# GpSimd makes the low parts of a weight strip, and of half of the second matrix, in one operation each

## The chip, the cores and the metric
The kernel runs on one core of one Trainium2 chip. The metric is the device time of one execution in microseconds (us), the lower the better. The core has five engines that this case speaks of: TensorE (PE) multiplies matrices, with its weight loads shown apart (PEld); VectorE (DVE), ScalarE (ACT) and GpSimd (POOL) work elementwise; SyncE (SP) here only issues DMAs. Each engine takes its own instructions in their order, and the kernel's author has set every wait between them by hand, with semaphores.

## The reference
Attention with a sliding window and four sink positions gives x (1536 tokens of 512). A first mixture of experts sends each token to one of eight experts. A second one, where this change lies, sends every token through all eight and adds them up with weights:

```python
for e in range(E):                     # E = 8, x: 1536x512, w1: 512x1024, w2: 1024x512
    h = np.maximum(x @ w1[e], 0.0)
    ye = h @ w2[e]
    out += P[:, e:e + 1] * ye
```

P are the gate's probabilities, balanced in eight rounds by rows and by columns (Sinkhorn).

## The kernel before, in words
Everything is computed in float32 to nearly full precision, though TensorE multiplies rounded numbers (fp32r). So every operand is split into a high part (rounded) and a low part (what the rounding left), and each product becomes three matmuls: high by high, high by low, low by high.

The first product of the second layer is made by Winograd's form of Strassen's scheme: the tokens' two halves and w1's rows and columns make 2x2 blocks, and seven products (P1, P6, P7, P2, P5, P4, P3, in that order) take the place of eight. For w1 this needs seven operand blocks of 256 numbers per partition: four that come from memory and sums of them. One such set of seven, 128x1792 numbers, is a *strip*. An expert has four strips (p = 0..3), kept in two buffers.

An expert's work is four *units* (u = 0..3). In a unit TensorE makes `up(e,u,0)` and `up(e,u,1)`, the first products for the two strips of the pair on one quarter of the tokens' columns (line 1995, 7 products of 6 matmuls of 384 columns each), and then `down(e,u)`, the second product (line 2020, 72 matmuls of 512 columns). Two units use the same pair of strips and the same half of w2 (`hu` = 0 or 1); here such two units are called a *half*. A half is then 2 x (up, up, down).

What the other engines do for it:

- GpSimd, for each half, in this order (`split_half`): for each of two strips four sums (lines 726 to 734), then, when ScalarE has rounded them, the low parts of the strip (line 739); then the low parts of half of w2, 128x2048 numbers in four chunks of 512 (line 746). The next strip's four sums stand behind these in its queue, and so do the next half's.
- ScalarE rounds a strip in two pieces (line 935) and w2 in four chunks (line 944). The four chunks are set between the steps of `up_evacuate` for the first up of the half: after the copy of P1's result, after the high part of block c11 (line 964), after c22's (line 970), and after c21's (line 974). Then come c12's high part (line 978) and the next up.
- VectorE (`up_finish`), for each up: u2 (line 1490), u3 (line 1497), the low part of c11, then c22 (line 1503), c21 (line 1509), the low part of c22, c12 (line 1514), and the low parts of c21 and c12. All low parts of the hidden values are line 1485; c11's reads the result bank `ps`, the other three read t_u3, t_c21 and t_u2 in SBUF. After a down it adds six output tiles to the accumulator (line 1525, reads `ps` and `acc`).

TensorE's waits inside an up: P6 of an up waits for the u2 of the up before, P4 (the sixth product) for this up's u3, P3 for its c22. A down waits for the low parts of w2 and for those of the hidden values. `up(e,u,j)` with even u waits for its strip.

At the start of the second layer the tokens' rows are read back, VectorE makes sums of them (`x2_combine`, lines 1435 to 1438, four operations a tile, all operands in SBUF), TensorE transposes, ScalarE rounds and VectorE makes the low part (line 1443, reads `ps`). During units 1 and 2 of the first expert VectorE also carries Sinkhorn's rounds (lines 1449 to 1460); lines 1451 and 1460 scale the table `mix` in SBUF, and TensorE adds up its columns (line 1958).

The loop over experts 1 to 7 is one code for all; expert 0 is written out ahead of it.

Of the kernel before, what the change touches and what calls it, by code (L numbers as in the profile page):

```python
# [8 lines left out]
ALU = mybir.AluOpType  # L9
# [9 lines left out]
def attention_moe_moe(nc, q, k, v, n_sink, window, modality_id, w_gate1, modality_bias, w1a, w2a,  # L19
# [37 lines left out]
    with ctx:  # L57
        def sem(name):
            return ctx.enter_context(nc.semaphore(name))
# [4 lines left out]
        def at(name, shape, dt, offset):  # L64
            return nc.alloc_sbuf_tensor_at(name, shape, dt, offset=BASE + offset)
# [174 lines left out]
        OPS = 7  # L240
# [10 lines left out]
        w1_raw = at("w1_raw", [PART, 2, OPS, 256], f32, R0 + 136 * KB)  # L251
        w1_lo = at("w1_lo", [PART, 2, OPS, 256], f32r, R0 + 136 * KB)
        w1_hi = at("w1_hi", [PART, 2, OPS, 256], f32r, R0 + 150 * KB)
        w2_raw = at("w2_raw", [PART, 4, DM], f32, R0 + 164 * KB)
        w2_hi = at("w2_hi", [PART, 4, DM], f32r, R0 + 172 * KB)
        w2_lo = at("w2_lo", [PART, 4, DM], f32r, R0 + 180 * KB)
# [116 lines left out]
        w1_split = sem("w1_split")  # L373
        w2_loaded = sem("w2_loaded")
        w2_rounded = sem("w2_rounded")
        w2_split = sem("w2_split")
# [202 lines left out]
        def _(pool):  # L579
# [142 lines left out]
            def split_w1(e, p):  # L722

                j, k = p % 2, e * 4 + p
                pool.wait_ge(w1_loaded[j], e * 64 + 32 * (p // 2 + 1))
                pool.tensor_tensor(w1_raw[:, j, OP_S1, :], w1_raw[:, j, OP_S3, :], w1_raw[:, j, OP_A22, :], ALU.add) \  # L726
                    .then_inc(w1_summed, 1)
                pool.tensor_tensor(w1_raw[:, j, OP_S3, :], w1_raw[:, j, OP_A11, :], w1_raw[:, j, OP_S3, :], ALU.subtract) \
                    .then_inc(w1_summed, 1)
                pool.wait_ge(w1_summed, e * 16 + (4 * p + 1))  # L730
                pool.tensor_tensor(w1_raw[:, j, OP_S2, :], w1_raw[:, j, OP_S1, :], w1_raw[:, j, OP_A11, :], ALU.subtract) \
                    .then_inc(w1_summed, 1)
                pool.wait_ge(w1_summed, e * 16 + (4 * p + 3))
                pool.tensor_tensor(w1_raw[:, j, OP_S4, :], w1_raw[:, j, OP_A12, :], w1_raw[:, j, OP_S2, :], ALU.subtract) \  # L734
                    .then_inc(w1_summed, 1)

                pool.wait_ge(w1_rounded, e * 8 + (2 * p + 2))
                for o in range(OPS):
                    last = pool.tensor_tensor(w1_lo[:, j, o, :], w1_raw[:, j, o, :], w1_hi[:, j, o, :], ALU.subtract)  # L739
                last.then_inc(w1_split, 1)  # L740

            def split_w2(e, hu):

                for c in range(4):
                    pool.wait_ge(w2_rounded, e * 8 + (4 * hu + c + 1))
                    last = pool.tensor_tensor(w2_lo[:, c, :], w2_raw[:, c, :], w2_hi[:, c, :], ALU.subtract)  # L746
                last.then_inc(w2_split, 1)

            def split_half(e, hu):
                split_w1(e, 2 * hu)  # L750
                split_w1(e, 2 * hu + 1)
                split_w2(e, hu)
# [1325 lines left out]
```

## Time and profile before
| | |
|---|---|
| median of 3 runs | 1405.94 us (1405.76 to 1407.05) |
| the profiled execution, its own time | 1408.68 us |
| its span, first to last instruction | 1406.9 us |
| PE busy | 1377.3 us, 98% |
| DVE busy | 705.2 us, 50% |
| ACT busy | 450.7 us, 32% |
| POOL busy | 411.4 us, 29% |
| mean granted TensorE clock | 0.990 of full speed |

The span is 1.8 us shorter than the time of its own execution, which holds what lies before the first and behind the last instruction. Busy times are sums over the whole program; which engine sets the end in a stage is read from what waits for what there. In the rows, a name without its number stands for all parts of a tensor: `h_lo<-t_u,h_hi` writes h2_lo from t_u2 or t_u3 and h2_hi, `w_lo` is w1_lo (128x256) or w2_lo (128x512).

### The profile page before, as it was taken

To read this page: it belongs to the slowest core of one execution; us is meant where nothing else is said; L and a number is where in the kernel's file an instruction comes from. 1 tells how busy PE (TensorE), PEld (TensorE's weight loads), DVE (VectorE), ACT (ScalarE), POOL (GpSimd) and SP (SyncE) were. 2 spreads that over 40 slices of the span, in tenths; PEclk is the share of its full clock that TensorE was granted. 3 is DMA by queue.
4 is the path that set the end of the run, shared out by engine and by line. 5 is a ranking of instruction groups with operands and counts; after the bars stand their busy time and mean duration, and the time that the engine had idled before them with its cause. 6 is when DMAs were issued, how large, how long until landed. Compare 5 with 4: busy or idle time off the path is not lost.

```text
span 1406.9 us, 21704 instructions
## 1 busy us (share of the span) xinstructions
PE 1377.3 (98%) x7527; PEld 1227.1 (87%) x7528; DVE 705.2 (50%) x1289; ACT 450.7 (32%) x867; POOL 411.4 (29%) x607
## 2 busy tenths in 40 slices
PE   8999989999799999999999999999999999999999
PEld 7999678888788888899998889999888899988888
DVE  7887572142464644444554444455444445544444
ACT  5887431242143432223131222323222222322221
POOL 2111022222430523325051432506143241605330
PEclk9999999999989999999999999999999999999999
DMA  6441352121301010101110101011101010110101
GB/s 131 90 101 44 137 212 102 45 75 38 135 31 31 30 31 31 31 31 30 45 45 30 30 30 30 30 45 45 30 30 30 30 30 32 36 48 33 30 31 59
DMA packets 95519, 73.85 MB, mean 52 GB/s; under 512 B 43248, under 2 KB 76016, under 8 KB 95472
## 3 DMA queue, kind: packets, MB, share of 16 engines
q1 hardware_dynamic: 90016, 65.32, 15.1%
q0 software_dynamic: 2416, 7.87, 1.7%
q8 instruction: 28, 0.46, 0.1%
q10 hardware_dynamic: 3040, 0.06, 0.1%
q14 instruction: 19, 0.16, 0.0%
HBM read 62.74 MB, written 10.49 MB: 52 GB/s over the span
## 4 chain that ended last, share of the span: by engine, by line
PE 92%; DVE 3%; SPq 1%; DMA 1%; ACT 1%; issue 1%; POOL 1%; POOLq 0%; DVEq 0%; ACTq 0%
PE ps L2020 37%; PE ps L1995 32%; PE ps L1859 6%; PE ps L1881 5%; PE ps L1680 3%; PE ps L1640 1%; PE ps L1614 1%; PE ps L1868 1%; PE ps L1674 1%; PE ps L1626 1%; PE ps L1793 1%; PE ps L1599 1%; PE ps L1928 1%; PE ps L1839 0%; SPq L465 0%
## 5 line engine op out<-in xcount | busy, mean ns | idle before, releaser
L1995 PE MATMUL ps<-x_hi,w_hi 128*128 128x384 f32 x896 | 301.9, 337 | 4.7 <-DVE x_lo L1443 3.8
L1995 PE MATMUL ps<-x_hi,w_lo 128*128 128x384 f32 x896 | 300.8, 336 | 0.0
L1995 PE MATMUL ps<-x_lo,w_hi 128*128 128x384 f32 x896 | 300.7, 336 | 0.0
L1525 DVE SCALAR_TENSOR_TENSOR acc<-ps,mix,acc 128x512 f32<-128x512 f32 x180 | 135.2, 751 | 329.1 <-PE ps L2020 329.1
L2020 PE MATMUL ps<-w_hi,h_hi 128*128 128x512 f32 x768 | 300.1, 391 | 0.0
L2020 PE MATMUL ps<-w_hi,h_lo 128*128 128x512 f32 x768 | 299.6, 390 | 0.0
L2020 PE MATMUL ps<-w_lo,h_hi 128*128 128x512 f32 x768 | 299.4, 390 | 0.0
L739 POOL TENSOR_TENSOR w_lo<-w_raw,w_hi 128x256 fp32r<-128x256 f32 x224 | 159.2, 746 | 89.5 <-ACT w_hi L935 89.5
L1995 PEld LDWEIGHTS ps<-x_hi,w_hi 128*128 128x128 f32 x896 | 169.1, 189 | 7.6 <-DVE x_lo L1443 4.2
L2020 PEld LDWEIGHTS ps<-w_hi,h_hi 128*128 128x128 f32 x768 | 144.1, 188 | 32.9 <-DVE h_lo L1485 5.0
L2020 PEld LDWEIGHTS ps<-w_hi,h_lo 128*128 128x128 f32 x768 | 144.1, 188 | 30.6
L1995 PEld LDWEIGHTS ps<-x_lo,w_hi 128*128 128x128 f32 x896 | 169.0, 189 | 1.2
L1995 PEld LDWEIGHTS ps<-x_hi,w_lo 128*128 128x128 f32 x896 | 169.0, 189 | 0.0
L2020 PEld LDWEIGHTS ps<-w_lo,h_hi 128*128 128x128 f32 x768 | 144.2, 188 | 27.7
L726 POOL TENSOR_TENSOR w_raw<-w_raw 128x256 f32<-128x256 f32 x32 | 23.7, 742 | 455.9 <-DMA w_raw<-in_moe_w_dram 448.4
L957 ACT ACTIVATE t_u<-ps 128x384 f32<-128x384 f32 x64 | 31.5, 492 | 311.8 <-PE ps L1995 311.8
L746 POOL TENSOR_TENSOR w_lo<-w_raw,w_hi 128x512 fp32r<-128x512 f32 x64 | 89.9, 1413 | 47.5 <-ACT w_hi L944 47.5
L935 ACT ACTIVATE w_hi<-w_raw 128x896 fp32r<-128x896 f32 x64 | 57.2, 942 | 126.7 <-POOL w_raw L734 126.7
L1485 DVE SCALAR_TENSOR_TENSOR h_lo<-t_u,h_hi 128x384 fp32r<-128x384 f32 x128 | 87.7, 685 | 6.1
L964 ACT ACTIVATE h_hi<-ps 128x384 fp32r<-128x384 f32 x64 | 31.5, 492 | 158.8 <-PE ps L1995 158.8
L613 POOL TENSOR_TENSOR hold_words<-ones 128x1 f32<-128x1 f32 x67 | 14.0, 208 | 232.8 <-DVE y_blk L1410 132.2
L1881 PE MATMUL ps<-wsplit,hT_hi 128*128 x224 | 69.0, 389 | 1.2 <-DVE hT_lo L1390 1.2
(279 smaller groups left out, 1784.7 us busy)
## 6 DMA issues: line engine op xcount, KB each, us to landing
w_raw<-in_moe_w_dram SPq DMA_DIRECT2D x64, 256.0 KB, 2.9
w_raw<-in_moe_w_dram SPq DMA_DIRECT2D x16, 1024.0 KB, 5.3
stage<-in_moe_w_dram SPq DMA_DIRECT2D x8, 1024.0 KB, 6.1
first_raw<-in_moe_w_dram SPq DMA_DIRECT2D x4, 1024.0 KB, 8.4
q_raw<-in_q_dram SPq DMA_DIRECT2D x12, 256.0 KB, 3.3
k_raw<-in_k_dram SPq DMA_DIRECT2D x12, 256.0 KB, 4.1
v_all<-in_v_dram SPq DMA_DIRECT2D x12, 256.0 KB, 4.4
x_rows_dram<-x_rows SPq DMA_DIRECT2D x12, 256.0 KB, 4.0
```

The lines of the kernel that those rows point to most:

```text
L739: last = pool.tensor_tensor(w1_lo[:, j, o, :], w1_raw[:, j, o, :], w1_hi[:, j, o, :], ALU.subtract)
L746: last = pool.tensor_tensor(w2_lo[:, c, :], w2_raw[:, c, :], w2_hi[:, c, :], ALU.subtract)
L935: act.activation(w_out[:, n * 896:(n + 1) * 896], w_raw[:, n * 896:(n + 1) * 896], ACT.Copy) \
L957: act.activation(t_u2[:, g % 2, :], ps[:, 0, 0:CT], ACT.Copy).then_inc(p1_copied, 1)
L964: act.activation(h2_hi[:, j, 0, 0, :], ps[:, 0, 0:CT], ACT.Relu).then_inc(c11_rounded, 1)
L1485: dve.scalar_tensor_tensor(out=h2_lo[:, j, a, b, :], in0=src, scalar=0.0, in1=h2_hi[:, j, a, b, :], op0=ALU.max, op1=ALU.subtract).then_in ...
L1525: dve.scalar_tensor_tensor(out=acc[:, m, :], in0=ps[:, 4 + t % 3, :], scalar=mix_flat[:, bass.ds(e + m * (E + 1), 1)], in1=acc[:, m, :], o ...
L1680: last = pe.matmul(ps[:, 7, l * D:(l + 1) * D], pT[:, par, (2 * l + t) * PART:(2 * l + t + 1) * PART], v_use[:, t, o:o + D], start=False, ...
L1859: last = pe.matmul(ps[:, fc, :], x_part[:, par, ks], wsplit[:, bass.ds(slot + (w_part + kc * F + fc * 512), 512)], start=(kc == 0 and n == ...
L1881: last = pe.matmul(ps[:, 4 + par, :], h_part[:, ks], wsplit[:, bass.ds(slot + (w_part + KD * F + kc * DM), DM)], start=(kc == 0 and n == 0 ...
L1995: last = pe.matmul(ps[:, bank, 0:CT], w_part[:, j, w, ks], x_part[:, x, k, cols], start=(opens and k == 0 and n == 0), stop=(k == 1 and n ...
L2020: last = pe.matmul(ps[:, 4 + t % 3, :], h_part[:, j, a, t // 3, ts], w_part[:, 2 * j + a, :], start=(j == 0 and a == 0 and n == 0), stop=( ...
```

## The change
In `split_w1` the seven subtractions of 128x256 become one of 128x1792 over the same bytes. In `split_w2` the four subtractions of 128x512, each with its own wait for the chunk that ScalarE rounds, become one of 128x2048 that waits for the fourth chunk. Nothing else is edited.

```diff
                 pool.wait_ge(w1_rounded, e * 8 + (2 * p + 2))
-                for o in range(OPS):
-                    last = pool.tensor_tensor(w1_lo[:, j, o, :], w1_raw[:, j, o, :], w1_hi[:, j, o, :], ALU.subtract)
-                last.then_inc(w1_split, 1)
+                pool.tensor_tensor(w1_lo[:, j, :, :].rearrange("p o n -> p (o n)"),
+                                   w1_raw[:, j, :, :].rearrange("p o n -> p (o n)"),
+                                   w1_hi[:, j, :, :].rearrange("p o n -> p (o n)"), ALU.subtract).then_inc(w1_split, 1)
 
             def split_w2(e, hu):
 
-                for c in range(4):
-                    pool.wait_ge(w2_rounded, e * 8 + (4 * hu + c + 1))
-                    last = pool.tensor_tensor(w2_lo[:, c, :], w2_raw[:, c, :], w2_hi[:, c, :], ALU.subtract)
-                last.then_inc(w2_split, 1)
+                pool.wait_ge(w2_rounded, e * 8 + (4 * hu + 4))
+                pool.tensor_tensor(w2_lo[:, :, :].rearrange("p c n -> p (c n)"),
+                                   w2_raw[:, :, :].rearrange("p c n -> p (c n)"),
+                                   w2_hi[:, :, :].rearrange("p c n -> p (c n)"), ALU.subtract).then_inc(w2_split, 1)
```

GpSimd's queue at the end of a half, in the loop over the experts, before (-) and now (+); w_raw, w_hi and w_lo are the raw, high and low parts of w1 in the 1792-wide rows and of w2 in the 2048-wide one, and a REGISTER_ALU row computes a semaphore's target:

```order
-L739 TENSOR_TENSOR w_lo<-w_raw,w_hi 128x256 x7
-L745 REGISTER_ALU
-L746 TENSOR_TENSOR w_lo<-w_raw,w_hi 128x512 x2
-L745 REGISTER_ALU
-L746 TENSOR_TENSOR w_lo<-w_raw,w_hi 128x512 x2
+L738 TENSOR_TENSOR w_lo<-w_raw,w_hi 128x1792
+L745 TENSOR_TENSOR w_lo<-w_raw,w_hi 128x2048
```

Eleven subtractions have become two; what stands ahead of them and behind them is the same. No instruction of another engine moves.

GpSimd's queue in the first half of the first expert, written out ahead of the loop, as it is now (before, the rows of lines 738 and 745 were `x7` of 128x256 and `x4` of 128x512); w_raw's rows are the sums, gmax is the maximum for the gate:

```order
L738 TENSOR_TENSOR w_lo<-w_raw,w_hi 128x1792
L726 TENSOR_TENSOR w_raw<-w_raw 128x256
L728 TENSOR_TENSOR w_raw<-w_raw 128x256
L731 TENSOR_TENSOR w_raw<-w_raw 128x256
L734 TENSOR_TENSOR w_raw<-w_raw 128x256
L738 TENSOR_TENSOR w_lo<-w_raw,w_hi 128x1792
L745 TENSOR_TENSOR w_lo<-w_raw,w_hi 128x2048
L756 ISA
```

The order here too is that of before; only the pieces are larger.

## Rows read from the trace of the kernel before
**Rows 1.** The page: busy time of TensorE and GpSimd.
```profile
PE 1377.3 (98%) x7527; PEld 1227.1 (87%) x7528; DVE 705.2 (50%) x1289; ACT 450.7 (32%) x867; POOL 411.4 (29%) x607
```
**Rows 2.** Busy time by stretch: length, engines, clock, DMA share, GB/s.
```profile
366.00:390.30 24.30, 14.64 (x115) 13.55 (x113) 13.87 (x16) 8.46 (x7) 13.61 (x18) 0.84 0.53 184
520.20:1402.00 881.80, 881.80 (x4435) 796.81 (x4434) 419.51 (x681) 220.76 (x394) 293.56 (x360) 1.00 0.11 35
```
**Rows 3.** Waits of weight loads from 520 us on: us in total, times, longest.
```profile
PEld ps L2020 <- DVE h_lo L1485: 4.7, 29, 0.2
```
**Rows 4.** Groups from 520 us on: busy us, mean ns of one, idle before.
```profile
L739 POOL TENSOR_TENSOR w_lo<-w_raw,w_hi 128x256 fp32r<-128x256 f32 x196 | 137.6, 738 | 75.6 <-ACT w_hi L935 75.6
L746 POOL TENSOR_TENSOR w_lo<-w_raw,w_hi 128x512 fp32r<-128x512 f32 x56 | 79.1, 1421 | 45.0 <-ACT w_hi L944 45.0
L1485 DVE SCALAR_TENSOR_TENSOR h_lo<-t_u,h_hi 128x384 fp32r<-128x384 f32 x114 | 78.3, 687 | 5.5
L1485 DVE SCALAR_TENSOR_TENSOR h_lo<-ps,h_hi 128x384 fp32r<-128x384 f32 x56 | 31.2, 558 | 49.7 <-ACT h_hi L964 49.7
```
**Rows 5.** Line 1525, whole program: duration ns min/median/max.
```profile
L1525 DVE SCALAR_TENSOR_TENSOR acc<-ps,mix,acc x180: 750/751/754, 492.1 to 1403.7; 128x512 f32<-128x512 f32 x180
```
**Rows 6.** GpSimd in one half: start us, us, what.
```profile
541.89 1.29 POOL L746 TENSOR_TENSOR w_lo<-w_raw,w_hi 128x512 fp32r<-128x512 f32 x1 [1.75 <-ACT w_hi L944]
543.56 3.06 POOL L746 TENSOR_TENSOR w_lo<-w_raw,w_hi 128x512 fp32r<-128x512 f32 x2 [0.38 <-ACT w_hi L944]
```
**Rows 7.** ScalarE, the same half.
```profile
543.91 0.61 ACT L944 ACTIVATE w_hi<-w_raw 128x512 fp32r<-128x512 f32 x1
544.51 0.53 ACT L978 ACTIVATE h_hi<-t_u 128x384 fp32r<-128x384 f32 x1
```
**Rows 8.** VectorE, the same half.
```profile
544.40 1.08 DVE L1485 SCALAR_TENSOR_TENSOR h_lo<-t_c,h_hi 128x384 fp32r<-128x384 f32 x1
545.40 1.64 DVE L1485 SCALAR_TENSOR_TENSOR h_lo<-t_u,h_hi 128x384 fp32r<-128x384 f32 x1
546.97 0.55 DVE L1490 TENSOR_TENSOR t_u<-ps,t_u 128x384 f32<-128x384 f32 x1
547.60 0.56 DVE L1497 TENSOR_TENSOR t_u<-ps,t_u 128x384 f32<-128x384 f32 x1
...
551.68 0.55 DVE L1485 SCALAR_TENSOR_TENSOR h_lo<-t_c,h_hi 128x384 fp32r<-128x384 f32 x1
```
**Rows 9.** TensorE, the same half: the first matmul of P4 and of the down.
```profile
548.92 0.33 PE L1995 MATMUL ps<-x_hi,w_hi 128*128 128x384 f32 x1
...
551.00 0.39 PE L2020 MATMUL ps<-w_hi,h_hi 128*128 128x512 f32 x1
```
**Rows 10.** GpSimd, copies in the attention (one operand a broadcast column).
```profile
L639 POOL TENSOR_TENSOR v_use<-v_all,ones 128x512 f32<-128x512 f32 x12 | 12.5, 1038 | 0.0
```
**Rows 11.** GpSimd, DVE and PE at the start of the second layer.
```profile
373.88 6.19 POOL L739 TENSOR_TENSOR w_lo<-w_raw,w_hi 128x256 fp32r<-128x256 f32 x7 [1.91 <-ACT w_hi L935]
...
375.07 0.95 DVE L1436 TENSOR_TENSOR y_rows<-y_rows 128x256 f32<-128x256 f32 x1
381.14 3.94 DVE L1443 TENSOR_TENSOR x_lo<-ps,x_hi 128x1792 fp32r<-128x1792 f32 x2
...
383.30 1.94 PE L1928 MATMUL ps<-ident,y_rows 128*128 128x128 f32 x8 [3.75 <-DVE x_lo L1443]
```
**Rows 12.** GpSimd, DVE and PE during Sinkhorn's rounds.
```profile
463.93 4.92 POOL L739 TENSOR_TENSOR w_lo<-w_raw,w_hi 128x256 fp32r<-128x256 f32 x7 [3.45 <-ACT w_hi L935]
473.73 4.91 POOL L739 TENSOR_TENSOR w_lo<-w_raw,w_hi 128x256 fp32r<-128x256 f32 x7 [1.90 <-ACT w_hi L935]
...
465.38 0.77 DVE L1460 SCALAR_TENSOR_TENSOR mix<-mix,col_sum 128x96 f32<-128x96 f32 x1
475.14 0.83 DVE L1460 SCALAR_TENSOR_TENSOR mix<-mix,col_sum 128x96 f32<-128x96 f32 x1
...
477.42 0.48 PE L1958 MATMUL ps<-mix,ones 128*128 128x117 f32 x2 [0.96 <-DVE mix L1451]
```

## The prediction
> **What bounds the kernel now.** I read the page's busy times first: TensorE is busy for 98% of the span, GpSimd for 29% [rows 1]. An engine at 29% gives nothing by being faster unless somebody waits for it, so next comes the view by stretches. From 520 us to 1402 us, 14 halves of the second layer, TensorE is busy in 881.8 of 881.8 us at full clock [rows 2]: there it alone sets the time. The list of waits names one thing for it in that stretch, 29 waits of 0.2 us for the last hidden low parts, and none for GpSimd [rows 3]. So the instructions that GpSimd saves are worth nothing in 63% of the span, and the question is what the new form does to others. For that I read the same group of VectorE instructions by form, and the timelines of three engines over one half.
>
> **A wait in the trace that no semaphore explains.** The low part of a hidden block is one instruction of 384 columns. In the form that reads the result bank it takes 558 ns on average; in the form that reads SBUF twice, 687 ns [rows 4]. In the half's timeline one such instruction takes 1.64 us, from 545.40 to 547.04, and the one before it 1.08 us, from 544.40 to 545.48; in the next up the same instruction, with GpSimd idle, takes 0.55 us [rows 8]. GpSimd's last two chunks run from 543.56 to 546.62 [rows 6]. The 1.64 us end 0.42 us after GpSimd's last chunk ended. So VectorE was held until a whole GpSimd instruction was over, and then ran. It goes the other way too: two chunks of 1.29 us take 3.06 us there, 0.48 us longer than 2.58, about what VectorE's work put between. The additions to the accumulator, which read only one large operand in SBUF, take 750 to 754 ns in all 180 cases, beside GpSimd or not [rows 5]. My reading: VectorE with both large operands in SBUF and GpSimd shut each other out, an instruction at a time. The length of the shut-out is then the length of GpSimd's instruction, and that is what the change makes four and seven times larger.
>
> The Trainium skill says it outright ("SBUF — State Buffer", section "Who interferes with whom"): a VectorE instruction with two SBUF inputs contends with a GpSimd instruction that reads SBUF, and whoever issues first has the ports "for the whole instruction". The trace agrees, with the 1.64 us against 0.55 us; that it holds for an instruction of 4 us is not shown by any row, and by this rule it would.
>
> **Durations of the new instructions.** A free chunk of 512 takes 1.29 us [rows 6] and a piece of 256 takes 0.738 us [rows 4], so 256 columns more cost 0.552 us, 2.16 ns a column. 2048 columns: 1.29 + 6 x 0.552 = 4.60 us. 1792: 1.29 + 5 x 0.552 = 4.05 us, where seven pieces took 4.92 us [rows 12]. Bounds for 2048: four free chunks, 5.16 us, from above; from below 4 x 1.038 = 4.15 us by the copy that has one full operand [rows 10]. I take 4.60, the line through two rows of the same operation.
>
> The same skill has a price ("GPSIMD Engine Reference", the table under "Reconciling with measured numbers"): 4497 ns for this operation on 2048 float32. No row here has it; by it each term below would be 0.1 us smaller.
>
> **w2 in one operation, step by step (14 halves in the loop and one before).** ScalarE ends the fourth chunk's rounding at 543.91 + 0.61 = 544.52 [rows 7]. VectorE's c21 low part has begun at 544.40, now with no chunk beside it, and ends 0.55 later, at 544.95. GpSimd's instruction has been waiting since 544.59 and gets in. VectorE's next one, c12's low part, can't come before: it needs c12's high part, ready at 544.51 + 0.53 = 545.04 [rows 7]. GpSimd then ends at 544.95 + 4.60 - 0.15 = 549.40; the 0.15 us is the start-up that a waiting instruction already has behind it (in before, 1.14 us lay between VectorE's end at 545.48 and GpSimd's end at 546.62, where a free chunk takes 1.29). Behind the held low part stand u2 and u3. From GpSimd's end to u3's took 546.62 to 548.16, 1.54 us [rows 6, 8]. So u3 is there at 550.94. TensorE needs it for P4, which now starts at 548.92 [rows 9]. It will wait 2.02 us, some 0.05 for the semaphore, and a start after a stall costs about 0.1 more: 2.2 us. What is late next: P3 needs c22, two VectorE instructions after u3, about 1.05 us, and P4 itself lasts 1.04 us, so nothing more comes of it. The down at 551.00 [rows 9] waits for w2's low parts, ready at 549.40; the 1.6 us of cover stay, and grow by the stall. The stall is not made up later, since TensorE has no other idle time in which to absorb it. 15 x 2.2 = 33 us. With 4.15 us it is 1.75 and 26 us, with 5.16 us 2.76 and 41 us. It would be nothing only if the instruction took under 2.6 us.
>
> **Strips in one operation, in the loop.** They run during a down, when VectorE only adds to the accumulator and isn't held [rows 5], and before the next up's first low part. The strip is ready 0.87 us earlier, but TensorE doesn't wait for it. Cost nothing, gain nothing; were that cover gone, each could cost up to 4 us.
>
> **Start of the second layer (+2.7 us).** The first strip's seven pieces start at 373.88, and VectorE's sums of token rows alternate with them: 0.95 us where one takes 0.42 alone [rows 11]. TensorE waits for the chain behind these sums, 3.75 us [rows 11]. Now VectorE is held from 374.7 until GpSimd's 4.05 us are over, about 378.2. Its eight sums still have to run, and GpSimd's next four sums fall among them: 4 x 0.85 + 4 x 0.45 = 5.2 us, 383.4 to 384, where VectorE came to its low part at 381.14 [rows 11]. That is 2.3 to 2.9; I take 2.7. Without any alternation it is 8 x 0.45, +0.7. The second strip holds four more sums that have 1 us to spare before u3: nothing.
>
> **Sinkhorn's stretch (+5.3 us).** The scaling at 465.38 comes into the strip that starts at 463.93 [rows 12]: held to 468.0 instead of 0.77 us in all, 2.2 us later, and TensorE's next column sum with it. The one at 475.14 comes into the strip at 473.73, whose end would be 477.8: 1.8 us, less 0.5 because the next scaling is now free. TensorE already waits for this chain, 0.96 us at 477.42 [rows 12], so it passes on. ScalarE and GpSimd give back up to 0.9. Then the half's w2 instruction holds c12's low part as above, 2.2, and a round of Sinkhorn stands in VectorE's queue between u2 and u3, so there is less slack, +0.5. The sum is 2.2 + 1.3 - 0.9 + 2.7 = 5.3; 3 to 8 with errors in where the pieces meet.
>
> **Sum.** 33 + 2.7 + 5.3 = 41 us on the profiled execution, 1408.68 to 1450, its span 1406.9 to 1448. The median before is 1405.94, 2.7 below the profiled time; the effect is a difference, so the forecast is 1405.94 + 41 = 1447 us. Its own range is 26 + 0.7 + 3 = 30 to 41 + 3.4 + 8 = 52: 1436 to 1458.
>
> **Rivals.**
> 1. *The hold is broken up.* GpSimd's instruction may let VectorE in between parts of its work. For it: no row shows a hold longer than the 1.3 us of one chunk. Against: the hold grew from 256 to 512 columns as the instruction did. Then nothing is late and TensorE's stretch stays as it is: within 1 us of before, 1406 us. 9%.
> 2. *Faster.* The same, and the start and Sinkhorn's stretch gain: VectorE's sums and scalings wait less than for a full piece now (some 0.4 us on each of seven sums, 3 us, and 0.5 on each of four scalings, 2 us), and the strip on the chain of waits at 463.93 is 0.87 us shorter. Together up to 6 us, 1400 us. It decides where a held VectorE instruction gets in after less than half a piece. 4%.
> 3. *VectorE goes first.* If both low parts of VectorE come ahead of GpSimd, the w2 instruction runs from about 545.5 to 550 beside instructions that read the bank and is over before the next low part at 550.64: no stall in the loop. It needs c12's high part 0.1 us earlier, at 544.95 instead of 545.04. Against: with both waiting at 545.4, GpSimd got in first [rows 6, 8]. Then only start and Sinkhorn remain, +6, 1412 us. 5%.
> 4. *The wait moves on.* If the long instruction were slower by the column (over 6.2 us), the down would wait for w2's low parts too, and the stall would be above 3.8 us: 1470 us. 2%.
>
> **How the numbers follow.** The forecast has 80%. All cases over 1408.8, that is, the forecast and rivals 3 and 4, make 87% slower; rival 1 and some of the others 9% same; 4% faster. The bound between these is 0.2%, 2.8 us, about what a measurement of this kernel can tell from no change. For 8 in 10 the range must reach a little beyond the own one, downward more, since an order of meetings that I misjudged would take stalls away: 1428 to 1459.
>
> **What would show it.** In the changed profile: POOL instructions of 1792 and 2048 columns of about 4.05 and 4.6 us (wrong over 5.2 or under 4.1); c12's low part in the first up of each half at about 5 us instead of 1.64; in the list of waits TensorE waiting for u3 (line 1497), 15 times, some 2 us each; TensorE's idle time from 520 us on about 30 us instead of none; the accumulator's additions at 751 ns still. If c12's low part stays below 2 us, the reading of the hold is wrong, and the forecast with it.

## The result and the profile after
The changed kernel took 1461.35 us, median of 5 runs (1459.78 to 1465.23), against 1405.94 us: 1.0388 of before, 95% interval 1.037 to 1.0405. It is slower by 55 us where I forecast 41, and lies 2 us above the range. That it gets slower was foreseen, by how much was not.

The page after, busy time by engine, beside [rows 1]:

```profile
PE 1396.9 (96%) x7527; PEld 1241.8 (85%) x7528; DVE 751.3 (51%) x1289; ACT 450.5 (31%) x867; POOL 369.0 (25%) x367
```

GpSimd is busy for 42 us less, and VectorE for 46 us more with the same 1289 instructions. These are the groups of the new instructions and of the hidden low parts in the changed kernel, over the whole program, to set beside [rows 4]; the third line, the forms of one source line, has duration ns min/median/max:

```profile
L738 POOL TENSOR_TENSOR w_lo<-w_raw,w_hi 128x1792 fp32r<-128x1792 f32 x32 | 129.6, 4050 | 95.1 <-ACT w_hi L935 95.1
L745 POOL TENSOR_TENSOR w_lo<-w_raw,w_hi 128x2048 fp32r<-128x2048 f32 x16 | 76.8, 4800 | 132.3 <-ACT w_hi L944 132.3
...
L1485 DVE SCALAR_TENSOR_TENSOR h_lo<-t_u,h_hi x128: 546/554/4755, 402.7 to 1441.1; 128x384 fp32r<-128x384 f32 x128
```

1792 columns take 4.05 us, as worked out. The 4.80 us for 2048 columns hold 0.2 us of waiting behind VectorE. The longest low part went from 1.64 to 4.755 us. Here is VectorE in one half, beside [rows 8]:

```profile
555.66 0.55 DVE L1485 SCALAR_TENSOR_TENSOR h_lo<-t_c,h_hi 128x384 fp32r<-128x384 f32 x1
556.33 4.75 DVE L1485 SCALAR_TENSOR_TENSOR h_lo<-t_u,h_hi 128x384 fp32r<-128x384 f32 x1
561.01 0.55 DVE L1490 TENSOR_TENSOR t_u<-ps,t_u 128x384 f32<-128x384 f32 x1
561.65 0.56 DVE L1497 TENSOR_TENSOR t_u<-ps,t_u 128x384 f32<-128x384 f32 x1
```

and GpSimd and TensorE in the same half, with the first matmul of P4, beside [rows 6, 9]:

```profile
555.87 4.81 POOL L745 TENSOR_TENSOR w_lo<-w_raw,w_hi 128x2048 fp32r<-128x2048 f32 x1 [8.55 <-ACT w_hi L944]
...
562.26 0.69 PE L1995 MATMUL ps<-x_hi,w_hi 128*128 128x384 f32 x1 [1.91 <-DVE t_u L1497]
562.74 0.53 PE L1995 MATMUL ps<-x_lo,w_hi 128*128 128x384 f32 x1
```

The order of meetings is the one of the prediction: c21's low part first (0.55 us), then GpSimd, then c12's low part until GpSimd is over, then u2, u3, P4. The 1.91 us of waiting ahead of P4 stand in all 14 halves of the loop. The last row also has something that I had not foreseen: the matmuls behind the wait take 0.53 us, where [rows 9] has 0.33.

The view by stretches says why. It has two stalls, what follows each, and the loop as a whole (length, engines, granted clock, DMA share, GB/s), beside [rows 2]:

```profile
560.35:562.20 1.85, 0.00 (x1) 0.00 (x0) 1.76 (x4) 0.00 (x0) 0.32 (x1) 1.00 0.30 24
562.20:565.60 3.40, 3.34 (x10) 3.34 (x11) 1.95 (x5) 0.94 (x2) 0.00 (x0) 0.51 0.78 283
819.80:821.80 2.00, 0.09 (x2) 0.01 (x1) 1.91 (x4) 0.00 (x0) 0.41 (x1) 1.00 0.49 31
821.80:826.00 4.20, 4.20 (x21) 3.77 (x22) 3.47 (x7) 1.58 (x3) 0.00 (x0) 1.00 0.62 235
560.00:1454.00 894.00, 867.30 (x4289) 781.20 (x4289) 440.08 (x663) 211.09 (x377) 242.63 (x144) 0.99 0.10 34
```

Behind the stall that ends at 562.26 the clock granted is half, 1.2 GHz instead of 2.4, for 3.4 us. Behind an equal stall that ends at 821.79 it stays full. In this profiled execution seven of the loop's 14 stalls are followed by such a stretch. TensorE is busy for 867.3 of the loop's 894 us; the 26.7 us that are left are the 14 stalls.

**Where the 52.7 us between the two profiled spans lie.** From the first to the last addition to the accumulator, before, [rows 5] has 492.1 to 1403.7; after:

```profile
L1525 DVE SCALAR_TENSOR_TENSOR acc<-ps,mix,acc x180: 749/751/754, 503.3 to 1456.4; 128x512 f32<-128x512 f32 x180
```

That is 911.6 and 953.1, 41.5 more for 14 halves. How long one half is can be read from the first matmul of P4 in one half and in the next; these two stand 64.10 us apart, with no half-speed stretch between them:

```profile
627.95 0.44 PE L1995 MATMUL ps<-x_hi,w_hi 128*128 128x384 f32 x1 [1.91 <-DVE t_u L1497]
692.05 0.44 PE L1995 MATMUL ps<-x_hi,w_hi 128*128 128x384 f32 x1 [1.91 <-DVE t_u L1497]
```

Before, a half took 61.94 us (P4 at 548.92 [rows 9] and at 610.86), so a half without a half-speed stretch became 2.16 us longer. One with it became 3.7 us longer (562.26 to 627.95 and its like). 14 x 2.16 = 30.2 and 7 x 1.54 = 10.8, together 41.0. The stretch ahead of it, from the first up to the first addition, grew from 101.7 to 109.9 us, +8.2. The one from the first layer's last block to the first up grew from 26.1 to 26.9, +0.8. The rest, 2.3 us, lies before the second layer, where the same instructions ran. The eleven profiled kernels of this study spread by 6 us there, and they fall in three groups by the time at half clock that TensorE had near 30 us: none in five of them (the first layer's last block at 360.7 to 361.0 us), 6.8 us in three, before among them (363.8 to 364.2), and 13.7 us in three, the changed kernel among them (366.3 to 366.6). Kernels with the merged strips stand in all three groups, so these 2.3 us are not put down to the change.

### The profile page after: what moved, and what is told of

Its sections match the earlier page's. It is cut to its first block and busy times, and to the rows that moved or that the text cites. A ratio compares the mean times of both kernels' runs of the same rounds, so it can differ in the third digit from the quotient of the medians.

```text
span 1459.6 us, 21436 instructions
## 1 busy us (share of the span) xinstructions
PE 1396.9 (96%) x7527; PEld 1241.8 (85%) x7528; DVE 751.3 (51%) x1289; ACT 450.5 (31%) x867; POOL 369.0 (25%) x367
## 5 line engine op out<-in xcount | busy, mean ns | idle before, releaser
L1995 PE MATMUL ps<-x_hi,w_hi 128*128 128x384 f32 x896 | 307.7, 343 | 35.6 <-DVE t_u L1497 31.8
L1995 PE MATMUL ps<-x_hi,w_lo 128*128 128x384 f32 x896 | 306.0, 341 | 0.0
L1995 PE MATMUL ps<-x_lo,w_hi 128*128 128x384 f32 x896 | 305.3, 341 | 0.0
L1995 PEld LDWEIGHTS ps<-x_lo,w_hi 128*128 128x128 f32 x896 | 172.3, 192 | 1.2
L1995 PEld LDWEIGHTS ps<-x_hi,w_lo 128*128 128x128 f32 x896 | 172.5, 192 | 0.0
L2020 PEld LDWEIGHTS ps<-w_hi,h_lo 128*128 128x128 f32 x768 | 144.5, 188 | 30.8
L738 POOL TENSOR_TENSOR w_lo<-w_raw,w_hi 128x1792 fp32r<-128x1792 f32 x32 | 129.6, 4050 | 95.1 <-ACT w_hi L935 95.1
L1485 DVE SCALAR_TENSOR_TENSOR h_lo<-t_u,h_hi 128x384 fp32r<-128x384 f32 x128 | 137.9, 1077 | 8.1
L745 POOL TENSOR_TENSOR w_lo<-w_raw,w_hi 128x2048 fp32r<-128x2048 f32 x16 | 76.8, 4800 | 132.3 <-ACT w_hi L944 132.3
```

The source lines that it names most:

```text
L738: pool.tensor_tensor(w1_lo[:, j, :, :].rearrange("p o n -> p (o n)"), w1_raw[:, j, :, :].rearrange("p o n -> p (o n)"), w1_hi[:, j, :, :]. ...
L745: pool.tensor_tensor(w2_lo[:, :, :].rearrange("p c n -> p (c n)"), w2_raw[:, :, :].rearrange("p c n -> p (c n)"), w2_hi[:, :, :].rearrange ...
L1485: dve.scalar_tensor_tensor(out=h2_lo[:, j, a, b, :], in0=src, scalar=0.0, in1=h2_hi[:, j, a, b, :], op0=ALU.max, op1=ALU.subtract).then_in ...
L1995: last = pe.matmul(ps[:, bank, 0:CT], w_part[:, j, w, ks], x_part[:, x, k, cols], start=(opens and k == 0 and n == 0), stop=(k == 1 and n ...
L2020: last = pe.matmul(ps[:, 4 + t % 3, :], h_part[:, j, a, t // 3, ts], w_part[:, 2 * j + a, :], start=(j == 0 and a == 0 and n == 0), stop=( ...
```

## The experiments
Each kernel is the changed one but for the edit shown, unless said otherwise. The kernel before was run again beside them, with medians of 1408.6 to 1409.6 us, so the ratios count, and not the difference to 1405.94.

**1. The strips alone.** w2 stays in four chunks.

```diff
-                pool.wait_ge(w2_rounded, e * 8 + (4 * hu + 4))
+                for c in range(4):
+                    pool.wait_ge(w2_rounded, e * 8 + (4 * hu + c + 1))
+                    last = pool.tensor_tensor(w2_lo[:, c, :], w2_raw[:, c, :], w2_hi[:, c, :], ALU.subtract)
...
```

> Only the strips are made in one operation; w2 stays in four chunks with a wait each. Theory (the 2048-wide instruction holds VectorE and starves TensorE in each half): nothing is late in the loop, TensorE idles in none of its halves; only the start of the layer and Sinkhorn's stretch lose, 1 to 6 us in all, so 1407 to 1412 us. Rival (GpSimd's long strips matter as much, 32 of them): 1420 us or more.

The time is 1411.82 us, ratio 1.0032 (1.0014 to 1.005). In its profile TensorE is never idle from 520 to 1390 us, and the accumulator's stretch is that of before:

```profile
520.00:1390.00 870.00, 870.00 (x4385) 787.40 (x4384) 416.41 (x678) 221.73 (x395) 270.29 (x194) 1.00 0.10 34
...
L1525 DVE SCALAR_TENSOR_TENSOR acc<-ps,mix,acc x180: 750/751/754, 493.4 to 1405.1; 128x512 f32<-128x512 f32 x180
```

The theory holds: 28 instructions of 4.05 us in the loop cost nothing, since nothing meets them there. What is lost lies ahead of the loop: the first up to the first addition took 105.8 us instead of 101.7.

**2. w2 alone.** The strips stay in seven pieces.

```diff
+                for o in range(OPS):
+                    last = pool.tensor_tensor(w1_lo[:, j, o, :], w1_raw[:, j, o, :], w1_hi[:, j, o, :], ALU.subtract)
...
```

> Only w2's half is made in one operation; the strips stay in seven pieces. Theory: all 14 stalls of 1.9 us behind u3 in the loop remain, with about as many stretches at half clock: 1452 to 1460 us. Rival (the strips matter): 1435 us or less.

The time is 1453.93 us, ratio 1.0323 (1.0295 to 1.0351). The loop has its 14 stalls of 1.9 us, and six of them are followed by half clock. The two parts come near the whole, 0.3% and 3.2% against 3.9% (3.7% if the changed kernel is set against before as it was run again).

**3. TensorE kept busy in the stall.**

```diff
                     if name == "P4":
+                        if not isinstance(e, int) and u % 2 == 0 and j == 1:
+                            keep_busy(14, 7)
                         pe.wait_ge(u3_made, e * 8 + (g + 1))
```

> The changed kernel, and in experts 1 to 7 TensorE transposes the identity 14 times into an unused bank (its result is not used) before it waits for u3 in the second up of a half, where it stands idle 1.9 us. Theory (the 14 us beyond my sum are stretches of 3.4 us at half clock behind about half of the stalls, 1.5 us each): the clock stays at full speed in the loop and the time falls by 9 to 13 us, to about 1450 us, while each half still is 2.2 us longer than before. Rival (the clock is not to blame, or falls all the same): 1458 to 1465 us.

The time is 1450.8 us, ratio 1.0299 (1.0262 to 1.0336), about 10 us under the changed kernel. The rows are the 14 transposes, the wait that is left, and P4's first matmuls (L1997 is line 1995 there), then the loop as one stretch, with its granted clock, and the accumulator:

```profile
559.91 1.69 PE L1689 MATMUL ps<-ident 128*128 128x128 f32 x14
561.99 0.45 PE L1997 MATMUL ps<-x_hi,w_hi 128*128 128x384 f32 x1 [0.39 <-DVE t_u L1497]
562.27 0.34 PE L1997 MATMUL ps<-x_lo,w_hi 128*128 128x384 f32 x1
...
560.00:1440.00 880.00, 874.60 (x4470) 789.80 (x4469) 438.94 (x661) 211.15 (x377) 242.62 (x144) 1.00 0.10 34
...
L1525 DVE SCALAR_TENSOR_TENSOR acc<-ps,mix,acc x180: 750/751/754, 503.0 to 1445.5; 128x512 f32<-128x512 f32 x180
```

P4 starts no earlier by this, but its matmuls take 0.34 us, and the loop has a granted clock of 1.00 and no half-speed stretch. The accumulator's stretch is 942.5 us, 30.9 over before: 14 x 2.2. So the 10.6 us that went are what the clock had cost, and what stays is the wait itself, of the size that was predicted. The shares are those of one profiled execution of each kernel; the medians differ by 10.6 us too, though the two kernels were not measured side by side.

**4. The same instruction, after VectorE's low parts.**

```diff
                 pool.wait_ge(w2_rounded, e * 8 + (4 * hu + 4))
+                pool.wait_ge(h2_split, e * 32 + (16 * hu + 4))
```

> The changed kernel, but GpSimd's 2048-wide instruction also waits until VectorE has made the fourth low part of the half's first up (c12's). Theory (the order in which the two meet decides, not the length by itself): VectorE goes first, GpSimd runs beside instructions that read the result bank, about 5 us in 545.5 to 550.2 of the profile before; no stall of 1.9 us in the loop: 1406 to 1414 us, at most 0.3 us a half lost. Rival (a long GpSimd instruction slows VectorE's reads of the bank too, or w2 then comes too late for the down): 1430 us or more.

The time is 1413.54 us, ratio 1.0036 (1.0019 to 1.0053). One half, VectorE and GpSimd (line numbers are one higher):

```profile
550.04 0.56 DVE L1486 SCALAR_TENSOR_TENSOR h_lo<-t_u,h_hi 128x384 fp32r<-128x384 f32 x1
551.06 0.56 DVE L1491 TENSOR_TENSOR t_u<-ps,t_u 128x384 f32<-128x384 f32 x1 [0.46 <-PE ps L1996]
552.01 0.56 DVE L1498 TENSOR_TENSOR t_u<-ps,t_u 128x384 f32<-128x384 f32 x1 [0.39 <-PE ps L1996]
...
550.68 4.61 POOL L746 TENSOR_TENSOR w_lo<-w_raw,w_hi 128x2048 fp32r<-128x2048 f32 x1 [9.66 <-DVE h_lo L1486]
```

GpSimd's instruction is issued 1.1 us later in the half than in the changed kernel, and the loop's 41 us are gone: the accumulator's stretch is 911.6 us. What stays over before lies ahead of the loop (108.2 us from the first up to the first addition). The free instruction takes 4.61 us (predicted 4.60). VectorE runs u2 and u3, which read the bank, beside it at 0.56 us. So the cause is neither the length alone nor the start after the fourth rounding, but the meeting of the two.

**5. One operand in the bank.** Stale numbers are read, so these low parts are wrong.

```diff
-                rest(0, 1, u2, c12_rounded)
+                rest(0, 1, u2 if begin or j == 1 or u % 2 else ps[:, 4, 0:CT], c12_rounded)
```

> The changed kernel, but in experts 1 to 7, in the first up of a half, c12's low part reads the result bank 4 (stale numbers) in place of t_u2: the same operation of the same size with one operand in SBUF instead of two; these low parts are wrong. Theory (VectorE is held only where both large operands lie in SBUF): it takes 0.56 us beside the 2048-wide instruction instead of 4.75, u2 and u3 follow in time, and the loop has no stall: 1411 to 1420 us (start and first expert keep theirs). Rival (any VectorE instruction behind GpSimd's start is held, or GpSimd's length acts through its own lateness): 1455 us or more.

The time is 1419.52 us, ratio 1.0071 (1.0046 to 1.0096). VectorE and GpSimd in one half:

```profile
558.66 0.56 DVE L1485 SCALAR_TENSOR_TENSOR h_lo<-ps,h_hi 128x384 fp32r<-128x384 f32 x1
559.68 0.56 DVE L1490 TENSOR_TENSOR t_u<-ps,t_u 128x384 f32<-128x384 f32 x1 [0.46 <-PE ps L1995]
...
558.19 4.82 POOL L745 TENSOR_TENSOR w_lo<-w_raw,w_hi 128x2048 fp32r<-128x2048 f32 x1 [8.55 <-ACT w_hi L944]
```

The operation is the same, issued 0.47 us behind GpSimd's, and takes 0.56 us instead of 4.75. This is the sharpest of the tests: nothing but the place of one operand was changed, and the loop is that of before (accumulator 505.6 to 1417.3, 911.7 us). The 10 us that the kernel still loses lie ahead of the loop, where the edit isn't made (111.0 us from the first up to the first addition, and 28.0 us before it).

**6. Four chunks, all behind the fourth rounding.**

```diff
+                for c in range(4):
+                    last = pool.tensor_tensor(w2_lo[:, c, :], w2_raw[:, c, :], w2_hi[:, c, :], ALU.subtract)
...
```

> The changed kernel with w2 in four instructions of 512 again, but all behind the wait for the fourth rounding. Theory (the length of one instruction matters, not that it starts late): c12's low part waits for one chunk, about 1.6 us in all as before, no stall in the loop: 1406 to 1413 us. Rival (the late start matters, w2 is late for the down or VectorE is held by the queue of chunks): 1440 us or more.

The time is 1410.04 us, ratio 1.0018 (1.0001 to 1.0036). The low part takes 1.43 us and the chunks together 5.55:

```profile
546.10 1.43 DVE L1485 SCALAR_TENSOR_TENSOR h_lo<-t_u,h_hi 128x384 fp32r<-128x384 f32 x1
...
545.63 5.55 POOL L746 TENSOR_TENSOR w_lo<-w_raw,w_hi 128x512 fp32r<-128x512 f32 x4 [8.60 <-ACT w_hi L944]
```

GpSimd's work is longer and as late as in the changed kernel, and TensorE doesn't wait for it: the accumulator's stretch is 911.6 us. VectorE gets in after the first chunk.

**7 and 8. 1536 and 1024 columns.** The pieces (a, b) are (0, 1), (1, 4) and (0, 2), (2, 4).

```diff
+                for a, b in ((0, 1), (1, 4)):
+                    pool.wait_ge(w2_rounded, e * 8 + (4 * hu + b))
+                    last = pool.tensor_tensor(w2_lo[:, a:b, :].rearrange("p c n -> p (c n)"),
...
```

> The changed kernel with w2 in two instructions, 512 behind the first rounding and 1536 behind the fourth. Theory (stall = instruction minus 2.6 us): 1536 columns take 3.5 us, so 14 stalls of 0.8 to 1.0 us, 1.0 to 1.1 with the restart; 1424 to 1430 us if the clock doesn't fall, up to 12 us more if it does. Rival (a step and not a slope): as the changed kernel, or as before.

> The changed kernel with w2 in two instructions of 1024, behind the second and the fourth rounding. Theory: 1024 columns take 2.4 us, below the 2.6 us that VectorE has to spare before P4: no stall in the loop or one under 0.1 us, 1406 to 1413 us. Rival: half the effect of 2048, 1430 us.

With 1536 columns the time is 1431.67 us, ratio 1.0156 (1.0121 to 1.019), and with 1024 it is 1416.79 us, ratio 1.0065 (1.0042 to 1.0087). The first rows are the held low part, the wait before P4 and the accumulator with 1536; then come the held part, GpSimd and the accumulator with 1024 (line numbers two higher):

```profile
551.43 3.65 DVE L1487 SCALAR_TENSOR_TENSOR h_lo<-t_u,h_hi 128x384 fp32r<-128x384 f32 x1
...
556.25 0.45 PE L1997 MATMUL ps<-x_hi,w_hi 128*128 128x384 f32 x1 [0.81 <-DVE t_u L1499]
...
L1527 DVE SCALAR_TENSOR_TENSOR acc<-ps,mix,acc x180: 749/751/753, 498.4 to 1425.2; 128x512 f32<-128x512 f32 x180
```

```profile
548.42 2.31 DVE L1487 SCALAR_TENSOR_TENSOR h_lo<-t_c,h_hi 128x384 fp32r<-128x384 f32 x1
...
547.91 2.40 POOL L746 TENSOR_TENSOR w_lo<-w_raw,w_hi 128x1024 fp32r<-128x1024 f32 x1 [0.30 <-ACT w_hi L946]
...
L1527 DVE SCALAR_TENSOR_TENSOR acc<-ps,mix,acc x180: 749/751/753, 495.4 to 1410.6; 128x512 f32<-128x512 f32 x180
```

The stretches are 926.8 and 915.2 us, so a half grew by 1.09 us and by 0.26; with 2048 it is 2.16. The instruction of 1536 columns takes 3.71 us in the trace, about 3.5 without the 0.2 us that it waits behind VectorE. From there to 2048 columns it grows by 1.1 us and the half by the same. TensorE's wait is the instruction less 2.7 us both times (4.61 and 1.91, 3.5 and 0.81). The rival, a step, falls. No half-speed stretch follows the waits of 0.8 us in the loop; the total is 2 us above the 1424 to 1430 that I expected without one. With 1024 the total missed my 1406 to 1413 by 4 us, in part because before itself took 1409.6 beside it. I had not seen that the first piece, behind the second rounding, holds c22's low part (1.35 us) and so lets GpSimd's second piece in ahead of c21's. TensorE's weight loads then wait for u3 14 times, at most 0.3 us each, and the loop is 3.6 us longer. The first up to the first addition took 107.6 us there, 5.9 over before; which meetings with Sinkhorn's rounds make that up I did not take apart.

**9. A version that beats both.** The kernel before, with this in `split_w1`:

```diff
                 pool.wait_ge(w1_rounded, e * 8 + (2 * p + 2))
+                if isinstance(e, int) and p == 0:
+                    pool.wait_ge(x2_combined, 3)
```

> The kernel before, and GpSimd's very first strip waits until VectorE has made the sums of the first three token tiles, so that the two don't alternate there. Theory (each of the seven sums from 375 us on waits 0.43 us for a piece of 256): VectorE comes to its low part 3 us earlier, and the stretch from the first layer's last block to the first up falls from 26.1 to 23 to 24 us: 1403 to 1405 us where before has 1406, within what can be measured only just. Rival (GpSimd's strip, now 4 us later, becomes the bound of the first up, or the rows' loading does): that stretch stays or grows.

The time is 1402.97 us, ratio to before 0.9965 (0.995 to 0.9981): a third of a per cent faster, with the whole interval under 1. The rows are two of VectorE's sums, GpSimd's first strip and TensorE's first up (line numbers two higher), to set beside [rows 11]:

```profile
376.64 0.42 DVE L1438 TENSOR_TENSOR y_rows<-y_rows 128x256 f32<-128x256 f32 x1
377.09 0.43 DVE L1439 TENSOR_TENSOR comb_a<-y_rows 128x256 f32<-128x256 f32 x1
...
380.22 4.84 POOL L741 TENSOR_TENSOR w_lo<-w_raw,w_hi 128x256 fp32r<-128x256 f32 x7 [6.19 <-DVE comb_a L1440]
...
387.69 0.44 PE L1997 MATMUL ps<-x_hi,w_hi 128*128 128x384 f32 x1 [3.81 <-DVE x_lo L1445]
```

The sums take 0.42 us instead of 0.83 to 0.95, and GpSimd's seven pieces 4.84 instead of 6.19. The stretch from the first layer's last block (366.27 here) to the first up is 21.4 us, where before has 26.1: 4.7 less, more than the 2 to 3 that I expected. VectorE comes to its low part 3.2 us earlier, which is what the theory said. The other 1.5 us is TensorE's transposes there, which ran at full clock (eight in 1.06 us, where [rows 11] has 1.94). Whether that clock comes with the edit or by chance, one profile of each can't tell.

## Why the prediction missed
The forecast was 14.4 us short, 41 where 55.4 were measured. By the stretches above, the loop is 10.7 us over its part of the sum (41.5 against 14 x 2.2 = 30.8), the start 1.9 under, the first expert 0.7 over, 2.3 us come from ahead of the second layer, and 2.7 us from setting the changed kernel against a median of 1405.94 where the profiled execution of before took 1408.68. The last two are not put down to the change; against before as it was run again, the changed kernel is slower by 52 to 53 us. So whether the time lies 2 us above the range or inside it hangs on these 5 us. The 10.7 us that the sum lacked in the loop do not, and the step that lacked them is named below.

- *The reading of the hold* was right: an instruction at a time, either way, only with both large operands in SBUF. Runs 4, 5 and 6 change the meeting, the operand's place and the length, one each, and each takes the stall away.
- *Durations* were right: 4.60 and 4.05 us predicted, 4.61 and 4.05 measured. The Trainium skill's price for 2048 columns, which the prediction sets beside them ("GPSIMD Engine Reference", "Reconciling with measured numbers"), would have been 0.11 us short.
- *15 stalls of 2.2 us* were right: 2.16 to 2.2 a half, the one before the loop, which ends at 410.38, with the same 1.91 us. Their bounds rested on one us of stall for each us of instruction, and run 7 shows that slope.
- *The step that failed* is "so nothing more comes of it". I listed what is late next, P3 and the down, and did not list TensorE's clock, though the stall is idle time of TensorE and [rows 2] shows a clock of 0.84 in the one stretch before with such idle time. Seven stretches at half clock in the loop cost 7 x 1.54 = 10.8 us; run 3 took them away and nothing else, and the loop fell by 10.6. Another lies behind the stall of 3.15 us that ends at 496.59, in the first expert. With that term the sum would have been 41 + 11 = 52, 1458 us, at the edge of my range. That half of the stalls would be followed by it could not be read from the trace of before.
- *The strips in the loop* at nothing: right (run 1).
- *Start* predicted at +2.7, measured +0.8. Counted from the last block, VectorE came to its low part 1.9 us later (18.85 instead of 16.91 us), a little under the 2.3 to 2.9 of the working. Of these, 1.2 us came back, since the 14 transposes that took 3.3 us at half clock before took 2.1 at a better one: again the clock, with the other sign. In five other profiles with the merged strips the same stretch was 27.8 to 28.0, and in run 2, whose strips are those of before, it was 26.8 instead of 26.1. So the cost of the start is known to within about 1 us only. The 3.4 us that the upper bound of the range takes for the start stand nowhere in its working, whose own upper end is 2.9.
- *First expert*, 2.2 + 5.3 = 7.5 predicted, 8.2 measured, with that eighth stretch in it. The held scalings are there, 2.70 and 2.75 us instead of 0.77 and 0.83:

```profile
470.33 2.70 DVE L1460 SCALAR_TENSOR_TENSOR mix<-mix,col_sum 128x96 f32<-128x96 f32 x1
481.51 2.75 DVE L1460 SCALAR_TENSOR_TENSOR mix<-mix,col_sum 128x96 f32<-128x96 f32 x1
```

- *Rivals.* A hold that is broken up (1 and 2) falls by the 4.75 us. VectorE going first (3) did not happen by itself; forced in run 4, it gave 1413.5, near the 1412 of its sum. w2 late for the down (4) did not happen.

## What to carry to other kernels
Before GpSimd's instructions are merged, look in the trace for VectorE instructions whose duration varies at a fixed size. Here the longest case minus the usual one was the wait for a GpSimd instruction, 1.09 us, and merging four chunks made it 4.20 us. Between short pieces on GpSimd, VectorE gets in. If they must be merged, make GpSimd wait until VectorE's instructions with two operands in SBUF are through, as run 4 does. And when a sum ends in idle time of a TensorE that ran without a pause, allow for the clock: here it added a third to the stalls themselves.

## What the runs showed of the hardware beyond that
- Idle time of 1.9 us in TensorE was followed by 3.4 us at half the clock in 7 of 14 equal cases in the changed kernel, 1.54 us lost each, and in 6 of 14 in run 2. Idle times of 0.8 us (run 7) and 0.4 us (run 3) never were. Why the clock falls behind one of two equal stalls and not behind the other was not tried.
- GpSimd's subtraction of two float32 operands takes 1.29, 2.40, 4.05 and 4.61 us for 512, 1024, 1792 and 2048 columns: 2.16 ns a column and 0.18 us fixed. Seven pieces of 256 took 4.92 us, so merging saves 18% of GpSimd's time on a strip, and here that was worth nothing.
- The Trainium skill ("SBUF — State Buffer", section "Who interferes with whom") says that a VectorE instruction with two inputs in SBUF and a GpSimd instruction that reads SBUF contend for an exclusive lock. This case agrees, up to a GpSimd instruction of 4.61 us: a VectorE operation of 0.55 us took 4.75, and with one operand in the bank 0.56 (run 5).
